# V in thirds over 128 partitions, ScalarE's copies swapped, and the last weight splits moved behind the lists

## The chip, the cores and the metric

The kernel runs on one core of one Trainium2 chip. The metric is the device time of one execution in microseconds (us), as the median of several runs; lower is better.

## The reference

Three layers in one kernel, all float32: an attention layer over 2 x 8 heads of 768 tokens, a top-2 mixture of 8 experts over the 1536 tokens, and a top-1 mixture with a skip. The change touches what is computed in the attention layer and between it and the first mixture's experts.

```python
def _attn_ref(q, k, v):                      # each (2, 8, 768, 64)
    block, window = (32, 16)
    k_sum = k.reshape(B, H, nb, block, D).max(axis=3)
    v_sum = v.reshape(B, H, nb, block, D).mean(axis=3)
    scores_l = scale * np.matmul(q, k.transpose(0, 1, 3, 2))
    mask_l = np.abs(pos[:, None] - pos[None, :]) < window
    scores_s = scale * np.einsum('bhsd,bhnd->bhsn', q, k_sum) + np.log(block)
    scores_all = np.concatenate([np.where(mask_l, scores_l, -1e9), scores_s], axis=-1)
    a = softmax(scores_all)
    return np.matmul(a, np.concatenate([v, v_sum], axis=2))

def _moe_ref(x, w_gate, w_noise, noise, w1, w2):
    noisy_logits = x @ w_gate + np.log1p(np.exp(x @ w_noise)) * noise
    top2 = np.argpartition(-noisy_logits, 2, axis=1)[:, :2]
    top2_w = softmax(noisy_logits[top2])
    for e in range(8):
        for k in range(2):
            mask = top2[:, k] == e
            out[mask] += top2_w[mask, k, None] * (np.maximum(x[mask] @ w1[e], 0.0) @ w2[e])
```

## The kernel before

The program is written engine by engine: SP issues the loads, PE (TensorE) multiplies, ACT (ScalarE), DVE (VectorE) and POOL (GpSimd) do the rest, each in an order written out by hand, with semaphores between them. An engine that waits holds everything behind it in its own order.

**Attention** works on 12 tiles of 128 tokens (6 per batch, `NT`), each in two steps of four heads (`NG = 2`, so 24 steps, `STEPS`). For a tile PE makes the scores of both steps (`scores`, L714) against a window of 96 keys and the 24 block maxima of the keys. DVE scales and masks them and takes the row maximum (`softmax`, L1562 and L1567). ACT takes the exponentials (`exponentials`, L1071). PE transposes them (`turn_p`, L725), ACT copies the transposed probabilities out of PSUM (`empty_pt`, L1078), and PE multiplies them with a window of V and the 24 block means of V (`times_v`, L742). DVE normalises a finished tile (`normalise`, L1574 to L1581) into `x_sb`, POOL stores it (`store_x`, L1324), PE transposes it (`do_job` of an "x" job, L676), ACT copies that (`empty_job`, L486, `xt_a`), and PE forms the router's logits (`router_logits`, L754). Every engine walks over the same step number s with lags: transposes at s - 2, P times V at s - 3, the x transposes at even steps from 6. On ACT a step is this, so that the copy of a step's probabilities stands at the beginning of the next step, behind the x copy (`PV_LAG = 3`):

```python
if 0 <= s - PV_LAG < STEPS:
    empty_pt(s - PV_LAG)
if 0 <= s - 1 < STEPS:
    exponentials(s - 1)
for job in at_step.get(s, []):
    empty_job(eng, job)
```

The first `times_v` of a tile waits until DVE has written `x_sb` of the tile before (semaphore `s_x`), since the accumulators are reused. The scores of a tile wait until the masks of the tile before are done (`s_masked`).

**Block means of V.** Raw V of a batch lies as 96 partitions of 8 tokens, in two halves of four tokens. POOL sums the first half (`value_sums`, L1316 and L1318), DVE the second (`value_sum`, L1550 and L1553), each in two additions; PE multiplies both with the matrix `mean` (L680, four matmuls, each shown twice by the profile). ACT copies the result to `vsum`, and POOL copies it into each of the eight windows of V (L1346), in between its copies of key windows (`window_of_keys`, L1303).

**Weights.** A set of weights is 8 pieces of 128 x 1024 numbers, loaded into `stage` by SP from the seventh tile on (`PIECE_TILE = 6`). Every product in the experts uses the weight rounded (`w_hi`) and the rest (`w_lo`). For the first set POOL rounds all pieces (`round_first`, L1329); DVE takes the rest of pieces 0 to 3 between attention steps (`split_first`, L1598, `SPLIT_AT`), and POOL itself the rest of pieces 4 to 7 after its last store (L1356).

**Routing** runs on DVE (`route`, L1639 to L1738) behind attention: softplus noise, top two, ranks of the tokens in their experts, then one-hot lists that PE multiplies, and the index lists (`index_lists`, L1757 to L1763). Then `first_mixture` starts: DVE clears a few buffers (L1774 to L1778), PE waits for that, runs twelve matmuls on nothing (`keep_warm`, L694), transposes the first gathered tokens (L815), which POOL gathers by an indirect DMA (L1430), and starts the first expert (L846).

**SP's queue** before the first tile: identity, keys of batch 0 in four transfers, the first of six query chunks, V in two halves, then tile by tile the windows of V, with the other queries, keys and V of batch 1 in between. Queries lie in rows of 1 KB. The third transfer of V waits for a free buffer (`VR = 3`).

## Time and profile before

| | |
|---|---|
| median of 3 runs | 688.26 us (687.83 to 688.34) |
| the profiled execution | 688.8 us, of which the span in the profile is 686.9 us |
| PE busy | 629.4 us (92%) |
| DVE, ACT, POOL busy | 369.5 (54%), 293.2 (43%), 247.3 us (36%) |
| mean granted TensorE clock | 0.946 of full speed |
| first expert matmul (L846) | 140.67 us after the span's start |
| attention, to the last logits | 105.0 us |
| routing and lists on DVE | 105.7 to 130.7 us |

The span's clock starts at the first instruction. All times of rows are in us from there. Matmuls of float32 appear as two records each. A busy engine is not necessarily the one that sets the end; for that the last wait of each step has to be read.

### The profile page before, as it was taken

To read this page: it belongs to the slowest core of one execution; us is meant where nothing else is said; L and a number is where in the kernel's file an instruction comes from. 1 tells how busy PE (TensorE), PEld (TensorE's weight loads), DVE (VectorE), ACT (ScalarE), POOL (GpSimd) and SP (SyncE) were. 2 spreads that over 40 slices of the span, in tenths; PEclk is the share of its full clock that TensorE was granted. 3 is DMA by queue.
4 is the path that set the end of the run, shared out by engine and by line. 5 is a ranking of instruction groups with operands and counts; after the bars stand their busy time and mean duration, and the time that the engine had idled before them with its cause. 6 is when DMAs were issued, how large, how long until landed. Compare 5 with 4: busy or idle time off the path is not lost.

```text
span 686.9 us, 13569 instructions
## 1 busy us (share of the span) xinstructions
PE 629.4 (92%) x4063; PEld 559.7 (81%) x4063; DVE 369.5 (54%) x711; ACT 293.2 (43%) x534; POOL 247.3 (36%) x231
## 2 busy tenths in 40 slices
PE   6788881699999999999999999999699999999994
PEld 6476771499999999999999999997478888888883
DVE  4564778655363545436354544630755669467541
ACT  2354750443253444335244432524254666546531
POOL 2552618220361816336170633606013223222130
PEclk9777996599999999999999999999799999999998
DMA  8985697236182654829265482798186859667321
GB/s 267 289 239 187 183 332 250 59 86 211 52 217 84 167 165 87 258 52 235 81 171 154 99 248 52 171 320 196 27 262 236 275 159 347 183 197 236 80 46 16
DMA packets 59380, 119.79 MB, mean 174 GB/s; under 512 B 13541, under 2 KB 16869, under 8 KB 58929
## 3 DMA queue, kind: packets, MB, share of 16 engines
q1 hardware_dynamic: 41168, 94.33, 42.9%
q0 software_dynamic: 14304, 23.93, 16.6%
q10 hardware_dynamic: 3840, 0.73, 0.5%
q8 instruction: 31, 0.51, 0.3%
q14 instruction: 37, 0.30, 0.1%
HBM read 103.48 MB, written 23.50 MB: 185 GB/s over the span
## 4 chain that ended last, share of the span: by engine, by line
PE 83%; DVE 5%; DMA 5%; SPq 2%; issue 2%; ACT 1%; POOLq 0%; DVEq 0%; ACTq 0%; POOL 0%
PE bank L960 22%; PE bank L852 21%; PE bank L846 21%; DMA q_ring<-in_q 3%; PE bank L835 2%; PE bank L815 2%; PE bank L742 2%; PE bank L976 2%; PE bank L754 2%; PE bank L694 2%; DMA xg<-x_moe,ix_take 1%; PE bank L714 1%; PE bank L725 1%; PE bank L764 1%; SPq L518 1%
## 5 line engine op out<-in xcount | busy, mean ns | idle before, releaser
L1589 DVE TENSOR_TENSOR w_lo<-stage,w_hi x120 | 141.6, 1222 | 22.9 <-ACT w_hi L1085 21.5
L1085 ACT CAST w_hi<-stage x120 | 119.7, 1050 | 9.4 <-PE bank L960 9.2
L852 PE MATMUL bank<-unit_hi,w_hi 128*128 128x416 f32 x256 | 92.6, 362 | 0.0
L846 PE MATMUL bank<-tok_hi,w_hi 128*128 128x416 f32 x256 | 90.5, 354 | 0.6 <-DVE tok_lo L1797 0.6
L852 PE MATMUL bank<-unit_lo,w_hi 128*128 128x416 f32 x256 | 90.2, 352 | 0.0
L1845 DVE SCALAR_TENSOR_TENSOR unit_lo<-bank,unit_hi 128x416 fp32r<-128x416 f32 x64 | 37.9, 592 | 96.9 <-ACT unit_hi L1186 96.9
L846 PE MATMUL bank<-tok_hi,w_lo 128*128 128x416 f32 x256 | 89.7, 351 | 0.0
L852 PE MATMUL bank<-unit_hi,w_lo 128*128 128x416 f32 x256 | 89.7, 350 | 0.0
L1186 ACT ACTIVATE unit_hi<-bank 128x416 fp32r<-128x416 f32 x64 | 33.2, 519 | 129.7 <-PE bank L846 129.7
L1396 POOL DMA_INDIRECT x_more<-more_out,ix_put x32 | 51.9, 1621 | 41.8 <-DVE more_out L1816 26.3
L1408 POOL DMA_INDIRECT x_moe<-rows_out,ix_put x32 | 55.2, 1726 | 9.8 <-issue 9.8
L846 PE MATMUL bank<-tok_lo,w_hi 128*128 128x416 f32 x256 | 58.5, 350 | 0.0
L1376 POOL COPY ix_take<-take_ix 128x4 int32 (+1 forms) x8 | 1.5, 186 | 135.8 <-PE bank L815 135.8
L846 PEld LDWEIGHTS bank<-tok_hi,w_hi 128*128 128x128 f32 x256 | 48.0, 188 | 1.6 <-issue 1.0
L852 PEld LDWEIGHTS bank<-unit_hi,w_hi 128*128 128x128 f32 x256 | 48.1, 188 | 1.0
L852 PEld LDWEIGHTS bank<-unit_hi,w_lo 128*128 128x128 f32 x256 | 48.3, 188 | 0.5
L846 PEld LDWEIGHTS bank<-tok_hi,w_lo 128*128 128x128 f32 x256 | 48.1, 188 | 0.4
L852 PEld LDWEIGHTS bank<-unit_lo,w_hi 128*128 128x128 f32 x256 | 48.0, 188 | 0.4
L846 PEld LDWEIGHTS bank<-tok_lo,w_hi 128*128 128x128 f32 x256 | 47.9, 187 | 0.5
L960 PE MATMUL bank<-w_hi,ht_hi 128*128 128x512 f32 x112 | 46.7, 417 | 0.0
L960 PE MATMUL bank<-w_hi,xt_hi 128*128 128x512 f32 x112 | 45.6, 407 | 0.5 <-ACT xt_hi L1229 0.5
L960 PE MATMUL bank<-w_lo,ht_hi 128*128 128x512 f32 x112 | 44.3, 395 | 0.0
(165 smaller groups left out, 1101.7 us busy)
## 6 DMA issues: line engine op xcount, KB each, us to landing
stage<-in_moe_w SPq DMA_DIRECT2D x128, 512.0 KB, 5.4
v_win<-in_v SPq DMA_DIRECT2D x24, 198.0 KB, 6.3
v_raw<-in_v SPq DMA_DIRECT2D x4, 792.0 KB, 12.2
x_moe<-rows_out SPq DMA_DIRECT2D x12, 260.0 KB, 3.8
kt<-in_k SPq DMA_DIRECT2D x8, 384.0 KB, 10.6
q_ring<-in_q SPq DMA_DIRECT2D x6, 512.0 KB, 10.4
x_att<-x_sb POOLq DMA_DIRECT2D x12, 256.0 KB, 5.4
x_part<-x_moe SPq DMA_DIRECT2D x4, 768.0 KB, 8.0
```

Source lines behind the costliest of these rows:

```text
L694: eng.matmul(ps[:], w_hi[0][:, 0, 0:P], w_hi[0][:, 0, :], start=True, stop=True)
L742: last = eng.matmul(ps_heads[part, h, 0:HD + 1], pt_sb[:, s % 2, i, part], v_win[:, (2 * t + half) % WR, h * VD:(h + 1) * VD], start=True, ...
L754: last = eng.matmul(ps_gate[:, t * cols:(t + 1) * cols], xt_a[t % 2][:, i, :], wgate1[:, i, :], start=(i == 0), stop=(i == DK - 1), skip_g ...
L846: last = eng.matmul(ps_unit[f % 2][:, 0:W], w, x, start=(i == 0), stop=(i == len(mine) - 1))
L852: last = eng.matmul(ps_out[chunk][:, 0:W], w[:, WC // 2 + f, chunk * P:(chunk + 1) * P], h[:, f % UNITS, :], start=(f == 0 and i == 0), st ...
L960: last = eng.matmul(ps[:], *every[i], start=(i == 0), stop=(i == len(every) - 1))
L1085: eng.copy(piece(w_hi[n % SETS], j), stage[:, j, :]).then_inc(s_hi, 1)
L1186: eng.activation(unit_hi[:, f % UNITS, :], ps_unit[f % 2][:, 0:W], ACT.Relu)\
L1396: eng.indirect_dma_start(more_dram, bass.IndirectOffsetOnAxis(ap=ix_put[0:rows, t:t + 1], axis=0), more_out[0:rows, t, :], None, bounds_ch ...
L1408: eng.indirect_dma_start(x1_dram, bass.IndirectOffsetOnAxis(ap=ix_put[0:rows, t:t + 1], axis=0), rows_out[0:rows, t, :], None, bounds_chec ...
L1589: eng.tensor_tensor(piece(w_lo[n % SETS], j), stage[:, j, :], piece(w_hi[n % SETS], j).bitcast(F32), ALU.subtract)\
L1845: eng.scalar_tensor_tensor(unit_lo[:, f % UNITS, :], ps_unit[f % 2][:, 0:W], 0.0, unit_hi[:, f % UNITS, :].bitcast(F32), ALU.max, ALU.subt ...
```

## The change

It has seven parts.

1. Raw V of a batch is loaded as three thirds of 128 partitions with two tokens each (`VJ, VI = 3, 2`), into one buffer per batch, so that SP waits for none. Batch 1's thirds are issued in tile 3 instead of 3 and 4.
2. DVE sums all of it in one instruction of 1584 elements, at steps 0 and 8 instead of 1 and 10, ahead of the next step's `softmax`; POOL sums nothing. PE multiplies with three matrices, so six matmuls instead of four; for batch 1 one step earlier.
3. The constants that only the casts of step 2 use (512 of 896 columns) are loaded by SP behind V instead of by ACT ahead of everything.
4. The queries are laid out on the host so that a chunk is one row of 4 KB per partition. The second chunk moves behind the first four windows, the keys of batch 1 one tile forward.
5. ACT copies the transposed probabilities in their own step, ahead of that step's x or V copy. POOL works by tiles: both V window copies, then both key windows.
6. The weight pieces are loaded two tiles earlier (`PIECE_TILE = 4`). POOL rounds pieces 0 to 3, ACT pieces 4 to 7, at steps 20, 22, 24 and 26. DVE splits pieces 0 to 3 two steps earlier (17 to 23).
7. DVE splits pieces 4 to 7 behind `index_lists` and ahead of `first_mixture`; POOL splits none. These pieces are the first expert's second layer.

On DVE at the start, up to the second tile's first mask (`v_part` is the sum of V, `s_sb` the masked scores), before:

```order
L1562 SCALAR_TENSOR_TENSOR s_sb<-bank,c_early 128x480
L1567 TENSOR_REDUCE nmax<-s_sb 128x4
L1562 SCALAR_TENSOR_TENSOR s_sb<-bank,c_early 128x480
L1567 TENSOR_REDUCE nmax<-s_sb 128x4
L1550 TENSOR_TENSOR v_raw<-v_raw 96x1056
L1553 TENSOR_TENSOR v_part<-v_raw 96x528
L1562 SCALAR_TENSOR_TENSOR s_sb<-bank,c_early 128x480
```

and with the change:

```order
L1539 SCALAR_TENSOR_TENSOR s_sb<-bank,c_early 128x480
L1544 TENSOR_REDUCE nmax<-s_sb 128x4
L1530 TENSOR_TENSOR v_part<-v_raw 128x1584
L1539 SCALAR_TENSOR_TENSOR s_sb<-bank,c_early 128x480
L1544 TENSOR_REDUCE nmax<-s_sb 128x4
L1539 SCALAR_TENSOR_TENSOR s_sb<-bank,c_early 128x480
```

The sum moves from behind the second mask to between the first and the second.

On ACT in the third and fourth tile (`pt_sb` are the transposed probabilities, `xt_a` the transposed x, `p_sb` the exponentials), before:

```order
L1078 COPY pt_sb<-bank 120x512
L1071 ACTIVATE p_sb<-s_sb,nmax 128x120 x4
L486 COPY xt_a<-bank 128x512
L1078 COPY pt_sb<-bank 120x512
L1071 ACTIVATE p_sb<-s_sb,nmax 128x120 x4
```

and with the change:

```order
L1058 ACTIVATE p_sb<-s_sb,nmax 128x120 x4
L1065 COPY pt_sb<-bank 120x512
L482 COPY xt_a<-bank 128x512
L1058 ACTIVATE p_sb<-s_sb,nmax 128x120 x4
L1065 COPY pt_sb<-bank 120x512
```

The copy of the probabilities and that of x have changed places.

On DVE between the lists and the first mixture (`put_ix` is the last of the lists, the memsets are the first of `first_mixture`), before:

```order
L1759 TENSOR_TENSOR empty<-c_late,count 128x128
L1762 TENSOR_SCALAR empty<-empty,c_late 128x128
L1763 TENSOR_TENSOR put_ix<-bank,empty 128x128
L1774 MEMSET rows_out 128x3x8
L1775 MEMSET more_out 128x36
```

and with the change:

```order
L1737 TENSOR_TENSOR empty<-c_late,count 128x128
L1740 TENSOR_SCALAR empty<-empty,c_late 128x128
L1741 TENSOR_TENSOR put_ix<-bank,empty 128x128
L1576 TENSOR_TENSOR w_lo<-stage,w_hi 128x1024 x4
L1752 MEMSET rows_out 128x3x8
L1753 MEMSET more_out 128x36
```

The four splits that POOL made beside the routing now stand here. The diff, cut to its core:

```diff
     parts["mask"] = mask
-    mean = np.zeros((P, NSUM), np.float32)
-    mean[p[:VP], p[:VP] * VTOK // BLOCK] = 1.0 / BLOCK
+    mean = np.zeros((P, VJ, NSUM), np.float32)
+    for j in range(VJ):
+        mean[p, j, j * (NSUM // VJ) + p // (BLOCK // VI)] = 1.0 / BLOCK
     parts["mean"] = mean
...
-        at_step = {2: [("v", 0, hh) for hh in range(2)], 12: [("v", 1, hh) for hh in range(2)]}
-
-        POOL_SUMS = {0: 0, 8: 1}
-        DVE_SUMS = {1: 0, 10: 1}
-        KEY_MAXIMA = {5: (0,), 6: (1,), 7: (2,), 8: (3,)}
+        at_step = {2: [("v", 0, hh) for hh in range(2)], 11: [("v", 1, hh) for hh in range(2)]}
+
+
+        SUMS = {0: 0, 8: 1}
+        KEY_MAXIMA = {4: (0,), 5: (1,), 6: (2,), 7: (3,)}
...
-        PIECE_TILE = 6
+        PIECE_TILE = 4
...
                     eng.wait_ge(s_score, NG * 2 * (n - QR + 1))
-                eng.dma_start(q_ring[:, n % QR], q[b, :, :, part * QC:(part + 1) * QC])\
+                eng.dma_start(q_ring[:, n % QR], q[b, part].rearrange("p (i n) -> p i n", i=PAIRS))\
                    .then_inc(s_q[n % QR], 16)
-            def load_values(b, part):
-                if 2 * b + part >= VR:
-                    eng.wait_ge(s_vp[(2 * b + part - VR) % 2], (2 * b + part - VR) // 2 + 1)
-                eng.dma_start(raw_of(b, part)[:], v[b].rearrange("(p j) c -> p j c", j=VTOK)
-                              [:, VHALF * part:VHALF * (part + 1), :]).then_inc(s_rawv[b, part], 16)
+            def load_values(b):
+                for j in range(VJ):
+                    eng.dma_start(v_raw[b][:, j, :], v[b, j * VI * P:(j + 1) * VI * P]
+                                  .rearrange("(p i) c -> p (i c)", i=VI)).then_inc(s_rawv[b, j], 16)
...
                 n, j = divmod(g, PIECES)
-                if n == 1 and j < PIECES // 2:
+                if n == 1:
                     eng.wait_ge(s_first, j + 1)
-                elif n == 1:
-                    eng.wait_ge(s_first_down, j - PIECES // 2 + 1)
                 elif n > 1:
...
             load_queries(0)
-            for part in range(2):
-                load_values(0, part)
+            load_values(0)
+            eng.dma_start(c_early[:, casts - early:], const[:, casts:]).then_inc(s_casts, 16)
             for t in range(NT):
-                if t == 2:
-                    load_queries(1)
                 for w in (2 * t, 2 * t + 1):
                     load_window(w)
-                if t == 2:
+                if t == 1:
+                    load_queries(1)
                     load_keys(1)
                 elif t == 3:
-                    load_values(1, 0)
                     load_queries(2)
-                elif t == 4:
-                    load_values(1, 1)
+                    load_values(1)
                     load_queries(3)
...
                     land(1)
-            for j in range(NT - PIECE_TILE, PIECES):
-                load_piece(j)
             land(0)
...
                     cols = slice(job[2] * VC, (job[2] + 1) * VC)
-                    for part in range(2):
-                        last = eng.matmul(ps[0:NSUM, 0:VC], c("mean")[0:VP], v_part[part][:, cols],
-                                          start=(part == 0), stop=(part == 1))
+                    for j in range(VJ):
+                        last = eng.matmul(ps[0:NSUM, 0:VC], c("mean")[:, j, :], v_part[:, j, cols],
+                                          start=(j == 0), stop=(j == VJ - 1))
                 last.then_inc(s_tr, 1)
...
                             if e == 0:
-                                eng.wait_ge(s_first_down, PIECES // 2)
+                                eng.wait_ge(s_first, PIECES)
                             else:
...
-            eng.dma_start(c_early[:], const[:, early:nconst]).then_inc(s_const, 16)
+            eng.dma_start(c_early[:, 0:casts - early], const[:, early:casts]).then_inc(s_const, 16)
             eng.dma_start(c_late[:, P:early], const[:, P:early]).then_inc(s_late, 16)
...
+            def round_first(j):
+
+                eng.wait_ge(s_loaded, j + 1)
+                eng.copy(piece(w_hi[0], j), stage[:, j, :]).then_inc(s_fhi_down, 1)
+
+            ROUND_AT = (20, 22, 24, 26)
             eng.preload_act_table_set("natural_log_exp_and_others")
             for s in range(LAST + 1):
-                if 0 <= s - PV_LAG < STEPS:
-                    empty_pt(s - PV_LAG)
                 if 0 <= s - 1 < STEPS:
                     exponentials(s - 1)
+                if 0 <= s - TURN_LAG < STEPS:
+                    empty_pt(s - TURN_LAG)
                 for job in at_step.get(s, []):
                     empty_job(eng, job)
+                if s in ROUND_AT:
+                    round_first(PIECES // 2 + ROUND_AT.index(s))
             eng.wait_ge(s_gt[0], NT)
...
-            def value_sums(b):
-
-                eng.wait_ge(s_rawv[b, 0], 16)
-                if b:
-                    for hh in range(2):
-                        eng.wait_ge(s_tr, job_at["v", b - 1, hh] + 1)
-                tokens = raw_of(b, 0)
-                eng.tensor_tensor(tokens[:, 0:2], tokens[:, 0:2], tokens[:, 2:4], ALU.add).then_inc(s_vadd, 1)
-                eng.wait_ge(s_vadd, b + 1)
-                eng.tensor_tensor(v_part[0][:], tokens[:, 0, :], tokens[:, 1, :], ALU.add)\
-                   .then_inc(s_vp[0], 1)
+            def sums_beside(w):
+
+                b = w // NWIN
+                for hh in range(2):
+                    wait_job(eng, ("v", b, hh))
+                if w >= WR:
+                    eng.wait_ge(s_pv, NG * ((w - WR) // 2 + 1))
+                eng.tensor_copy(v_win[0:NSUM, w % WR], vsum[b][:]).then_inc(s_vw, 1)
...
-            STORE_LAG, ROUND = 5, 14
-            AHEAD = WKR
-            for w in range(AHEAD):
+            ROUND = 6
+            for w in range(WKR):
                 window_of_keys(w)
-            for w in range(BATCH * NWIN):
-                b = w // NWIN
-                if w in POOL_SUMS:
-                    value_sums(POOL_SUMS[w])
-                if w + AHEAD < BATCH * NWIN:
-                    window_of_keys(w + AHEAD)
-                if w % NWIN < WR:
-                    for hh in range(2):
-                        wait_job(eng, ("v", b, hh))
-                    if w >= WR:
-                        eng.wait_ge(s_pv, NG * ((w - WR) // 2 + 1))
-                    eng.tensor_copy(v_win[0:NSUM, w % WR], vsum[b][:]).then_inc(s_vw, 1)
-                if w >= STORE_LAG and w % 2:
-                    store_x((w - STORE_LAG) // 2)
-                if ROUND <= w < ROUND + PIECES and w % 2 == 0:
-                    round_first((w - ROUND) // 2)
+            for t in range(NT):
+                for w in (2 * t, 2 * t + 1):
+                    if w % NWIN < WR:
+                        sums_beside(w)
+                for w in (2 * t + WKR, 2 * t + WKR + 1):
+                    if w < BATCH * NWIN:
+                        window_of_keys(w)
+                if t >= 2:
+                    store_x(t - 2)
+                if ROUND <= t < ROUND + PIECES // 2:
+                    round_first(t - ROUND)
             for t in (NT - 2, NT - 1):
                 store_x(t)
-            for j in range(PIECES // 2, PIECES):
-                round_first(j)
-                eng.wait_ge(s_fhi, j + 1)
-                eng.tensor_tensor(piece(w_lo[0], j), stage[:, j, :],
-                                  piece(w_hi[0], j).bitcast(F32), ALU.subtract).then_inc(s_first_down, 1)
...
-
-                eng.wait_ge(s_rawv[b, 1], 16)
+                for j in range(VJ):
+                    eng.wait_ge(s_rawv[b, j], 16)
                 if b:
...
                         eng.wait_ge(s_tr, job_at["v", b - 1, hh] + 1)
-                tokens = raw_of(b, 1)
-                eng.tensor_tensor(tokens[:, 0:2], tokens[:, 0:2], tokens[:, 2:4], ALU.add)\
-                   .then_inc(s_vadd_d, 1)
-                eng.wait_ge(s_vadd_d, b + 1)
-                eng.tensor_tensor(v_part[1][:], tokens[:, 0, :], tokens[:, 1, :], ALU.add)\
-                   .then_inc(s_vp[1], 1)
+                eng.tensor_tensor(v_part[:], v_raw[b][:, :, 0:VROW], v_raw[b][:, :, VROW:2 * VROW],
+                                  ALU.add).then_inc(s_vp, 1)
...
-                eng.wait_ge(s_fhi, j + 1)
-                for hh in range(2):
-                    eng.wait_ge(s_vp[hh], BATCH)
+                if j < PIECES // 2:
+                    eng.wait_ge(s_fhi, j + 1)
+                else:
+                    eng.wait_ge(s_fhi_down, j - PIECES // 2 + 1)
                 eng.tensor_tensor(piece(w_lo[0], j), stage[:, j, :],
...
-            SPLIT_AT = (19, 21, 23, 25)
+            SPLIT_AT = (17, 19, 21, 23)
             steps = [0]
...
                 if s == 2:
+                    eng.wait_ge(s_casts, 16)
                     eng.tensor_copy(before_b[:], c("before")).then_inc(s_cast, 1)
...
                     then(eng.tensor_copy(column_h[:], c("column")))
-                if s in DVE_SUMS:
-                    value_sum(DVE_SUMS[s])
+                if s in SUMS:
+                    value_sum(SUMS[s])
                 if s in SPLIT_AT:
...
             index_lists(0)
+            for j in range(PIECES // 2, PIECES):
+                split_first(j)
             first_mixture()
...
         laid[n] = pairs.reshape(BATCH, P, PAIRS, SEQ)
+    chunks = laid["q"].reshape(BATCH, P, PAIRS, QCHUNKS, QC).transpose(0, 3, 1, 2, 4)
+    laid["q"] = chunks.reshape(BATCH, QCHUNKS, P, PAIRS * QC)
     by_token = inputs["v"].transpose(0, 2, 1, 3)
```

## Rows read from the trace of the kernel before

**Rows 1.** The page: granted TensorE clock in 40 slices, tenths of full speed

```profile
PEclk9777996599999999999999999999799999999998
```

**Rows 2.** Windows: stretch, length, busy PE, PEld, DVE, ACT, POOL; clock, DMA share, GB/s

```profile
24.00:32.00 8.00, 6.72 (x76) 5.43 (x76) 2.11 (x6) 5.18 (x16) 5.77 (x11) 0.50 1.05 305
68.00:104.00 36.00, 31.19 (x517) 27.79 (x509) 25.00 (x45) 23.68 (x66) 14.66 (x24) 1.00 0.79 261
```

**Rows 3.** Timeline of PE in attention: start us, us, engine, line, operation [idle before]

```profile
15.42 1.05 PE L714 MATMUL bank<-k_win,q_ring 64*64 64x120 f32 x32
21.36 2.74 PE L680 MATMUL bank<-v_part,c_early 96*24 96x264 f32 x8 [3.43 <-DVE v_part L1553]
27.48 1.88 PE L714 MATMUL bank<-k_win,q_ring 64*64 64x120 f32 x32
39.06 1.59 PE L714 MATMUL bank<-k_win,q_ring 64*64 64x120 f32 x32 [1.01 <-DMA q_ring<-in_q]
...
61.10 3.71 PE L680 MATMUL bank<-v_part,c_early 96*24 96x264 f32 x8
67.65 1.05 PE L714 MATMUL bank<-k_win,q_ring 64*64 64x120 f32 x32
...
89.31 1.05 PE L714 MATMUL bank<-k_win,q_ring 64*64 64x120 f32 x32
```

**Rows 4.** Timeline of DVE in the routing, and of POOL beside it

```profile
105.74 1.22 DVE L1639 TENSOR_TENSOR score<-z_sp,noise_sb 128x96 f32<-128x96 f32 x1 [3.19 <-ACT z_sp L1105]
107.00 0.26 DVE L1641 TENSOR_TENSOR score<-bank,score 128x96 f32<-128x96 f32 x1
110.43 0.90 DVE L1673 CAST top_f<-top_ix 128x24 f32<-128x24 uint32 x1
111.76 2.28 DVE L1690 TENSOR_TENSOR mask_b<-hot 128x96 bf16<-128x96 f32 x1
113.97 1.00 DVE L1692 TENSOR_SCALAR first_f<-top_f 128x24 f32<-128x24 f32 x1
115.59 1.91 DVE L1707 TENSOR_SCALAR den<-den 128x12 f32<-128x12 f32 x1
...
111.38 2.56 POOL L1356 TENSOR_TENSOR w_lo<-stage,w_hi 128x1024 fp32r<-128x1024 f32 x1
```

**Rows 5.** Timeline of DVE, its sums of V

```profile
18.22 2.07 DVE L1550 TENSOR_TENSOR v_raw<-v_raw 96x1056 f32<-96x1056 f32 x1 [2.77 <-DMA v_raw<-in_v]
53.34 1.24 DVE L1550 TENSOR_TENSOR v_raw<-v_raw 96x1056 f32<-96x1056 f32 x1
54.62 0.70 DVE L1553 TENSOR_TENSOR v_part<-v_raw 96x528 f32<-96x528 f32 x1
```

**Rows 6.** Windows of the first transfers, columns as in rows 2

```profile
8.00:10.00 2.00, 2.00 (x16) 1.87 (x14) 1.65 (x3) 0.00 (x0) 0.27 (x1) 1.00 1.10 400
14.00:16.00 2.00, 2.00 (x36) 1.83 (x38) 1.41 (x3) 1.77 (x6) 0.63 (x1) 1.00 0.96 220
```

**Rows 7.** Timeline of PE, ACT and DVE in one attention tile at full clock

```profile
74.04 0.65 PE L725 MATMUL bank<-c_late,p_sb 128*120 128x128 f32 x4
...
77.86 0.69 PE L742 MATMUL bank<-v_win,pt_sb 120*64 120x65 f32 x16 [0.73 <-ACT pt_sb L1078]
...
76.73 0.59 ACT L486 COPY xt_a<-bank 128x512 f32<-128x512 f32 x1 [1.58 <-PE bank L676]
77.22 0.59 ACT L1078 COPY pt_sb<-bank 120x512 f32<-120x512 f32 x1
...
76.59 0.69 DVE L1581 TENSOR_TENSOR x_sb<-bank,rden 128x512 f32<-128x512 f32 x1
```

**Rows 8.** Timeline of DVE's splits of weights, and of PE's warm-up before the experts

```profile
83.87 1.81 DVE L1598 TENSOR_TENSOR w_lo<-stage,w_hi 128x1024 fp32r<-128x1024 f32 x1
89.29 1.22 DVE L1598 TENSOR_TENSOR w_lo<-stage,w_hi 128x1024 fp32r<-128x1024 f32 x1
...
131.52 4.61 PE L694 MATMUL bank<-w_hi 128*128 128x512 f32 x12 [2.24 <-DVE bank L1777]
```

31 lines of the change are left out of this document (13 added, 18 removed).

## The prediction

> **What bounds the kernel now.** I read the page's clock line and the windows of the first 150 us, then the chain of waits there, then the engines' timelines. The diff touches only what comes before the first expert layer, so all from the first expert matmul on is taken as unchanged and the sum lies in the first 141 us. TensorE (PE) carries the chain through attention. The reader is to see its two speeds: the clock line has 7 tenths in the three slices from 17 to 69 us [rows 1]; between 68 and 104 us PE has its full clock, in 24 to 32 us 0.50 of it, the lower of its two levels, 1.2 GHz [rows 2]. The starts of the score matmuls are the mileposts [rows 3]: second tile 15.42, third 27.48, fifth 39.06, eighth 67.65, twelfth 89.31 us. From the eighth on a tile takes (89.31-67.65)/4 = 5.42 us; the three from the fifth to the eighth took 28.59. Behind attention VectorE (DVE) computes the routing alone, and five of its small instructions take 0.9 to 2.3 us there, beside one of 96 elements at 0.26, while GpSimd (POOL) works on the weights [rows 4].
>
> **The change part by part.** The mileposts give the terms.
>
> *Start, up to the third tile.* DVE waits for V until 18.2 us [rows 5], and PE's V matmuls start at 21.36 [rows 3]. V (1.62 MB) passes in a stretch of 220 GB/s over 96 partitions; keys over 128 partitions came at 400 [rows 6]. At 220 V costs 7.4 us, at 400 4.1. The constants for the casts (0.26 MB, 0.7 us) also leave the stretch ahead of V. So V lands between 14.2 (both gains) and 18.2 (none); I take 15, near the fast row, because the thirds have the keys' 128 partitions. The new sum is one instruction of 1584 elements in place of 1056 and then 528, which take 1.24 and 0.70 us with POOL idle [rows 5], so 1.24 + 0.54 = 1.8. It now stands ahead of the second group's mask (0.7), and PE's second scores wait for that mask: 15 + 1.8 + 0.7 = 17.5. Scores, transposes and filler follow, 2.5 us as from 15.42 to the pause at 21.36 - 3.43 = 17.93 [rows 3]: 20.0. Then six V matmuls in place of four: a pass of four took 3.71 us at the low clock [rows 3], so six take 5.6 there and 2.8 at full. They end at 22.8 to 25.6. From their end (24.10) to the third scores 3.4 us passed before; the same gives 26.2 to 29.0. I take 26.8, nearer the full clock, since PE's pause is now only from about 15.5 to 17.5: **-0.7** (ends -2.1, with V at 14.2, and +4.7, with V at 18.2 and the low clock).
>
> *Third to fifth tile*, 11.58 us. With V faster and 0.8 MB less queued ahead of it, the third query chunk lands 4 us or more earlier, and PE's 1.01 us behind it go [rows 3]. The block maxima of the second keys come one step earlier and fill DVE, so I count no more: **-1.0** (0 to -2.0).
>
> *Fifth to eighth tile*, 28.59 us. Three tiles at 5.42 are 16.3, DVE's sum in front of a mask is 1.24 + 0.70 = 1.9 [rows 5], the V matmuls at full clock 1.9; that is 20.1, so 8.5 go to the low clock. Afterwards: three tiles at 4.9 (next term) 14.7, the sum 1.8, the V matmuls 2.8, together 19.3. The loss to the clock is what I know least: between 0 and the same 8.5. Of PE's pauses in this stretch the one behind queries goes and that behind ACT shrinks; that behind the sum stays. I take 6, nearer to before: 25.3, **-3.3** (-9.3 to -0.8).
>
> *The four tiles at full clock.* Here the swap on ScalarE (ACT) tells. PE's transposes of an even step are done at 74.04 + 0.65 = 74.69, but ACT empties them only at 77.22, because the copy of x stands first and waits for PE's own x transposes until 76.73; P times V starts at 77.86, having waited 0.73 [rows 7]. With the swap ACT is done before 76. What is late next is the normalisation: this P times V may not start before DVE has written x_sb, at 76.59 + 0.69 = 77.28. So it starts at 77.33, 0.53 earlier, and a tile takes 4.89. PE's own work is 5.42 - 0.73 = 4.7 a tile; DVE is busy 25.00 of 36 us, 3.8 a tile with its splits, ACT 23.68, 3.6 [rows 2], and 4.8 with a rounding if that takes what a split takes, 1.2 [rows 8]. All stay just under 4.89. Four tiles: **-2.1** (to 0, if roundings push an exponential).
>
> *The drain to the routing* has one more such wait, 0.5, and one of ACT's four roundings may stand before the last x copies, 0.3: **-0.2** (-0.5 to +0.8).
>
> *Routing.* The five slow instructions take 1.22 + 0.90 + 2.28 + 1.00 + 1.91 = 7.3 us. mask_b ends at 114.04 just as POOL's subtract of 111.38 does, at 113.94 [rows 4]: DVE is held behind POOL. With POOL idle they take at most 0.26 each, 1.3: **-6.0** (-6.4 to -5).
>
> *The splits behind the lists.* Four of DVE's 1024-element subtracts now stand between the lists and the memsets for which PE's twelve warm-up matmuls, at 131.52, wait [rows 8]. Nothing covers them; they in turn cover the gathers. Four by 1.22 are **+4.9** (4.5 to 7.2, the last by 1.81 each, the split that ran beside a POOL cast [rows 8]). POOL issues its four gathers just then; a gather's issue reads only a few indices, so I stay at 1.22. The next set's last four pieces load later for it, but their use is a whole expert round away.
>
> *At nothing:* queries in rows of 4 KB. The first queries, in rows of 1 KB, passed in the stretch of 400 GB/s [rows 6]. Thirds of 0.54 MB in place of halves of 0.81: DMA share is 0.96 to 1.10 with several transfers queued [rows 6], so a third costs its bytes. The Trainium skill (DMA: Bandwidth & Descriptors, "Rules for kernel authors") asks for 1 MiB or more per DMA and speaks against this part; with the page's fixed 2 us for the one transfer more, the sum would be an estimated -6.4. The share on these rows speaks against it.
>
> **Sum:** -0.7 -1.0 -3.3 -2.1 -0.2 -6.0 +4.9 = -8.4. The profiled execution took 688.8 us (span 686.9), so 680.4; it lies 0.5 above the median of the runs, 688.26, so I say **679.9**.
>
> **Rivals.**
> *The clock stays up.* Without the low level between the fifth and eighth tile that term is -9.3 and the time 679.9 - 6.0 = 673.9. For it: between 68 and 104 us PE was busy 31.19 of 36 us and kept its clock [rows 2], and 4.7 in 4.89 is denser. Against: DVE's sum still makes PE wait.
>
> *The clock falls as before.* The pause before the second scores brings the low level at the start (+2.2 on that term) and again later (-0.8 for -3.3): 679.9 + 4.7 = 684.6. For it: the low window of 24 to 32 us [rows 2] followed a pause of 3.43 us [rows 3].
>
> *The splits are held behind POOL's gathers,* 1.81 each: +2.3, 682.2. For it: mask_b and the 1.81 [rows 4, 8]. Against: no row shows a gather's issue holding DVE. The Trainium skill (SBUF — State Buffer, "Who interferes with whom") has this rule for a VectorE instruction with two SBUF inputs against a GpSimd one that reads SBUF, the later waiting for the whole of the earlier.
>
> *V is no faster in thirds* (18.2): 679.9 + 3.2 = 683.1.
>
> *The end on the other side: V is late for DVE's in-order queue.* The sum stands ahead of the second mask, so until all three thirds are in, masks, exponentials and PE stand, and each microsecond of V beyond 15 is one of the whole, at the low clock. That is the second rival's 684.6 plus the delay; it decides from V at 15 + 3.7 = 18.7 us, hardly later than now, and at 21 the kernel takes 690.6. For it: V is waited for as a whole before the second mask. Against: it was there at 18.2 behind more bytes.
>
> **How the numbers follow.** Forecast 0.40, clock up 0.16, clock as before 0.20, splits held 0.10, V no faster 0.08, V late 0.06. The range runs from the clock that stays up to the second rival with held splits or a late V in part: 673.5 to 686.0. A measurement of this kernel tells 0.2% (1.4 us) from no change. All but the last rival are faster by more, with a little off for two of them together: 0.90; within 0.2% 0.04; slower 0.06.
>
> **What would show it.** Right: V's sum on DVE starts at 14 to 16 us; third scores near 27, eighth near 63, twelfth near 82; a tile in 4.9 us with P times V waiting for DVE, not ACT; mask_b and den at 0.3 or less; four w_lo of 1.2 between put_ix and the memsets; the first expert matmul some 8 us earlier than before. Wrong: a V sum after 18 us; a clock of 0.50 through most of 22 to 60 us; w_lo behind the lists at 1.8; a tile above 5.2; a first expert matmul less than 3 us earlier.

## The result and the profile after

The changed kernel takes 678.92 us (median; 673.55 to 685.43 over 13 executions), the kernel before beside it 687.49. The medians differ by 8.6 us, where the prediction said 8.4; the ratio is 0.9892, 95% interval 0.9854 to 0.9931, which is 7.4 us. Both kernels vary by about 1% from one execution to the next, the slower ones mostly at a lower mean clock (0.952 to 0.972 for the changed kernel); the ratios leave out executions more than 1.5% above the fastest of the same kernel, such as one of 722.98 us among the six of warm_held. The profiled execution took 673.55 us (span 671.2) and is its quickest, so the 15.7 us between the two profiled spans are more than the change is worth at the median. Where a stretch is compared below, I also use the traces of experiments whose code is the same there.

The page's clock line of the changed kernel, against [rows 1]:

```profile
PEclk9999975999999999999999999999699999999998
```

Windows of the changed kernel (stretch, length, busy PE, PEld, DVE, ACT, POOL; clock, DMA share, GB/s), against [rows 2, 6]:

```profile
8.00:10.00 2.00, 0.48 (x5) 0.24 (x3) 1.54 (x2) 0.00 (x0) 0.72 (x3) 1.00 1.04 426
14.00:16.00 2.00, 0.68 (x7) 0.44 (x5) 1.94 (x2) 0.67 (x3) 0.00 (x0) 1.00 1.08 250
24.00:32.00 8.00, 6.30 (x141) 5.08 (x137) 6.13 (x11) 5.08 (x15) 7.47 (x15) 1.00 1.04 344
40.00:48.00 8.00, 6.10 (x99) 4.86 (x95) 5.99 (x10) 5.04 (x15) 2.22 (x6) 1.00 0.91 271
```

The clock is 1.00 throughout attention, up to 88 us. Before, it stood at 0.50 from 24 to 32 us [rows 2]. By SP's order the 250 GB/s from 14 to 16 us are windows of V, which go onto 96 partitions; V itself is in by then.

Timeline of PE: the mileposts, against [rows 3] (start, us, [idle before]):

```profile
16.58 1.05 PE L701 MATMUL bank<-k_win,q_ring 64*64 64x120 f32 x32 [1.90 <-DVE s_sb L1539]
19.02 2.85 PE L667 MATMUL bank<-v_part,c_early 128*24 128x264 f32 x12
24.60 1.05 PE L701 MATMUL bank<-k_win,q_ring 64*64 64x120 f32 x32 [0.17 <-issue]
34.90 1.38 PE L701 MATMUL bank<-k_win,q_ring 64*64 64x120 f32 x32 [0.78 <-DVE s_sb L1539]
41.89 1.05 PE L701 MATMUL bank<-k_win,q_ring 64*64 64x120 f32 x32 [1.64 <-DVE s_sb L1539]
54.56 1.05 PE L701 MATMUL bank<-k_win,q_ring 64*64 64x120 f32 x32
74.98 1.05 PE L701 MATMUL bank<-k_win,q_ring 64*64 64x120 f32 x32
```

Second, third, fifth, sixth, eighth and twelfth scores, with the V matmuls between the first two. Third 24.60 against 27.48, fifth 34.90 against 39.06, eighth 54.56 against 67.65, twelfth 74.98 against 89.31.

Timeline of DVE, then of POOL and PE behind the lists, against [rows 4, 5, 8]:

```profile
14.06 1.81 DVE L1530 TENSOR_TENSOR v_part<-v_raw 128x1584 f32<-128x1584 f32 x1 [0.68 <-DMA v_raw<-in_v]
91.69 0.26 DVE L1617 TENSOR_TENSOR score<-z_sp,noise_sb 128x96 f32<-128x96 f32 x1 [3.32 <-ACT z_sp L1100]
95.76 0.26 DVE L1668 TENSOR_TENSOR mask_b<-hot 128x96 bf16<-128x96 f32 x1
96.73 0.17 DVE L1685 TENSOR_SCALAR den<-den 128x12 f32<-128x12 f32 x1
109.83 0.29 DVE L1741 TENSOR_TENSOR put_ix<-bank,empty 128x128 int32<-128x128 f32 x1
110.27 4.63 DVE L1576 TENSOR_TENSOR w_lo<-stage,w_hi 128x1024 fp32r<-128x1024 f32 x4
...
111.54 2.01 POOL L1411 DMA_INDIRECT rows_in<-x_att,take_ix  x1 [0.30 <-issue]
116.11 0.95 POOL L1411 DMA_INDIRECT rows_in<-x_att,take_ix  x1 [0.30 <-issue]
...
115.23 4.70 PE L681 MATMUL bank<-w_hi 128*128 128x512 f32 x12 [6.53 <-DVE bank L1755]
124.48 0.45 PE L833 MATMUL bank<-tok_hi,w_hi 128*128 128x416 f32 x1 [0.58 <-DVE tok_lo L1775]
```

Routing and lists, from score to the end of put_ix, take 18.4 us against 24.9 (105.74 to 130.69). Then four splits in 4.63, and only then the warm-up. From the first expert matmul on the two traces differ little: 671.2 - 124.5 = 546.7 us here, 686.9 - 140.7 = 546.2 before.

### The profile page after: what moved, and what is told of

Read it like the earlier page. It is cut to its first block, busy times and chain, and to the rows that moved or that the text cites. A ratio compares the mean times of both kernels' runs of the same rounds, so it can differ in the third digit from the quotient of the medians.

```text
span 671.2 us, 13575 instructions
## 1 busy us (share of the span) xinstructions
PE 618.5 (92%) x4071; PEld 551.4 (82%) x4071; DVE 367.0 (55%) x713; ACT 297.0 (44%) x538; POOL 230.3 (34%) x219
## 4 chain that ended last, share of the span: by engine, by line
PE 85%; DVE 6%; DMA 3%; issue 2%; ACT 1%; SPq 1%; POOLq 0%; DVEq 0%; POOL 0%; ACTq 0%
PE bank L947 22%; PE bank L839 22%; PE bank L833 22%; PE bank L822 2%; PE bank L802 2%; PE bank L963 2%; PE bank L729 2%; PE bank L681 2%; PE bank L741 2%; PE bank L701 1%; PE bank L712 1%; DMA xg<-x_moe,ix_take 1%; DMA v_raw<-in_v 1%; PE bank L919 1%; DVE col_val L1728 1%
```

## The experiments

Each experiment was run beside the kernel before, on the same chip. Microseconds between two kernels are differences of these ratios times 686.

### Where DVE's routing instructions lost their time

**splits_pool**: the changed kernel with the last four subtracts on POOL.

```diff
 # POOL, behind the last store_x
+for j in range(PIECES // 2, PIECES):
+    eng.wait_ge(s_fhi_down, j - PIECES // 2 + 1)
+    eng.tensor_tensor(piece(w_lo[0], j), stage[:, j, :],
+                      piece(w_hi[0], j).bitcast(F32), ALU.subtract).then_inc(s_first_down, 1)
 # DVE, behind index_lists(0)
-for j in range(PIECES // 2, PIECES):
-    split_first(j)
```

> The changed kernel with the last four subtracts back on POOL, behind its last store of x, so beside the routing; the roundings stay on ACT. If POOL's subtract holds DVE's small instructions (the theory): those routing instructions that fall beside the four subtracts (some 2.6 us each, about 90 to 100 us) take 0.9 to 2.3 again, the stretch from the router's score to put_ix grows from 18.4 by 3 to 6 us, and the memsets come 4.6 sooner behind put_ix: the first expert matmul stands within -1.6 and +1.5 us of the changed kernel's. If the slow instructions of the kernel before came from something else (its POOL casts, or the place in the program): the stretch stays at 18.4, the first expert matmul comes 4.6 us sooner, and the whole takes some 674.5.

Measured: 683.28 us, ratio 0.9941 (0.9907 to 0.9975). Timeline of its POOL and DVE:

```profile
95.50 9.26 POOL L1344 TENSOR_TENSOR w_lo<-stage,w_hi 128x1024 fp32r<-128x1024 f32 x4
100.95 3.93 DVE L1624 TENSOR_TENSOR score<-z_sp,noise_sb 128x96 f32<-128x96 f32 x1 [6.39 <-ACT z_sp L1103]
104.91 0.26 DVE L1626 TENSOR_TENSOR score<-bank,score 128x96 f32<-128x96 f32 x1
```

POOL's four subtracts end at 104.76; DVE's 96-element score, which takes 0.26 alone, starts at 100.95 and ends at 104.88. All that follow are at full speed. So POOL holds DVE, and the whole growth of the stretch (22.1 us instead of 18.4) is this one instruction. The Trainium skill (SBUF — State Buffer, "Who interferes with whom") has the later instruction wait for the whole of the earlier one; here it waited for the next of the run as well, which started at 102.4. By the rows this kernel should equal the changed one: from score to the first expert matmul (133.80) it takes 32.9 us against 32.8, 3.7 lost in the routing and 3.6 won back behind the lists. The ratios put it 3.4 above, with intervals that overlap, and this rest I can't settle.

**before_splits**: the kernel before with the subtracts moved and POOL's roundings left.

```diff
 # POOL, behind the last store_x
 for j in range(PIECES // 2, PIECES):
     round_first(j)
-    eng.wait_ge(s_fhi, j + 1)
-    eng.tensor_tensor(piece(w_lo[0], j), stage[:, j, :],
-                      piece(w_hi[0], j).bitcast(F32), ALU.subtract).then_inc(s_first_down, 1)
 # DVE, behind index_lists(0)
+for j in range(PIECES // 2, PIECES):
+    split_first(j)
```

> The kernel before with this part of the change alone: the last four subtracts go from POOL to DVE, behind the lists; POOL keeps their four roundings beside the routing. If only POOL's subtracts held DVE: the five slow instructions fall to 0.3 or less, score to put_ix from 24.95 to some 19, four subtracts of 1.2 follow, and the first expert matmul comes 1 us or so sooner (time -1.3). If its casts hold DVE too: two or three of the five stay slow, and the whole is 1 to 3 us slower than the kernel before.

Measured: 686.9 us, ratio 1.0029 (0.9995 to 1.0064). The timeline of its POOL and DVE shows that the cast holds DVE as well, to the end of the run of four at 100.35:

```profile
96.37 3.98 POOL L1329 CAST w_hi<-stage 128x1024 fp32r<-128x1024 f32 x4
98.73 1.74 DVE L1637 TENSOR_TENSOR score<-z_sp,noise_sb 128x96 f32<-128x96 f32 x1 [3.19 <-ACT z_sp L1105]
118.90 4.63 DVE L1595 TENSOR_TENSOR w_lo<-stage,w_hi 128x1024 fp32r<-128x1024 f32 x4 [0.25 <-DVE put_ix L1761]
```

Four casts alone are over before the second slow instruction comes, so score to the end of put_ix takes 19.9 us, 5.0 less than before, and the subtracts give 4.4 back (memsets 4.83 behind put_ix, 0.45 before). **This part alone is worth nothing that can be measured.** The routing's gain and the splits' price nearly cancel: score to the first expert matmul takes 34.7 us against 34.9.

### What ScalarE's order carries

**swap_undone**: the changed kernel with the old order.

```diff
-if 0 <= s - 1 < STEPS:
-    exponentials(s - 1)
-if 0 <= s - TURN_LAG < STEPS:
-    empty_pt(s - TURN_LAG)
+if 0 <= s - PV_LAG < STEPS:
+    empty_pt(s - PV_LAG)
+if 0 <= s - 1 < STEPS:
+    exponentials(s - 1)
```

> The changed kernel with ScalarE's old order (probabilities of three steps back emptied first, then the exponentials, and the x copy ahead of the next emptying). If the swap carries what was predicted (0.53 a tile at full clock): the P times V matmuls of an even step again wait some 0.6 to 0.7 for ACT's pt_sb, the tiles from the eighth to the twelfth take 5.3 to 5.5 instead of 5.1 on average, and the whole is 3 to 6 us above the changed kernel (some 682 to 685). If DVE sets the pace of a tile anyway (rival): the tile stays at 5.1, the wait only changes its name, and the time is that of the changed kernel, 679 within a microsecond or two.

Measured: 687.4 us, ratio 1.0019 (0.9991 to 1.0047): the whole gain of the change is gone, more than the 682 to 685 expected. PE's waits in its timeline:

```profile
72.25 0.69 PE L729 MATMUL bank<-v_win,pt_sb 120*64 120x65 f32 x16 [0.73 <-ACT pt_sb L1065]
84.03 0.69 PE L729 MATMUL bank<-v_win,pt_sb 120*64 120x65 f32 x16 [1.67 <-ACT pt_sb L1065]
90.39 0.69 PE L729 MATMUL bank<-v_win,pt_sb 120*64 120x65 f32 x16 [1.67 <-ACT pt_sb L1065]
96.30 0.69 PE L729 MATMUL bank<-v_win,pt_sb 120*64 120x65 f32 x16 [1.67 <-ACT pt_sb L1065]
```

Tiles take 5.42 us again, the 0.73 of [rows 7], instead of 4.95. Three times the wait is 1.67: ACT's rounding of a weight piece, which takes 1.05, now stands between the x copy and the emptying that PE waits for (83.39). In its ACT timeline, ahead of the first of the three:

```profile
81.96 0.59 ACT L482 COPY xt_a<-bank 128x512 f32<-128x512 f32 x1 [1.56 <-PE bank L663]
82.44 1.05 ACT L1083 CAST w_hi<-stage 128x1024 fp32r<-128x1024 f32 x1
```

This P times V waits 0.26 in the changed kernel. Six waits of 0.73 are 0.47 longer, 2.8 us; three of 1.67 are 1.41 longer, 4.2: together an estimated 7.0 of the 8.7 lost. So the roundings on ACT are affordable only in the new order.

**before_swap**: the kernel before with that order alone (the same edit the other way round).

> The kernel before with ScalarE's new order alone. Undoing it in the changed kernel cost 8 us where 3 to 6 were expected, so the order may carry more than a wait of 0.53 a tile. If it does so by itself: the tiles from the eighth to the twelfth go from 5.42 to 4.9, those before them have shorter pauses and keep the clock more often, and the time falls by 4 to 8 us, to some 680. If it needs the other parts (V in time, the block maxima earlier; rival): the late tiles take 4.9, which is 2 us, the early ones stay as they were, and the time is 683 to 684.

Measured: 681.92 us, ratio 0.9950 (0.9912 to 0.9989), 3.4 us, between what its two expectations say. The eighth to the eleventh scores stand at 59.99, 64.94, 69.88 and 74.83, so 4.95 a tile, also without the other parts. Earlier tiles keep waits that the order doesn't touch, 3.10 us behind queries and 1.83 behind DVE's sum, with the clock at 0.50 from 40 to 44 us.

### V: partitions, and its place in DVE's queue

**v_96**: the changed kernel, each third as 96 and 32 partitions.

```diff
-for j in range(VJ):
-    eng.dma_start(v_raw[b][:, j, :], v[b, j * VI * P:(j + 1) * VI * P]
+for p0, p1 in ((0, 96), (96, P)):
+    for j in range(VJ):
+        eng.dma_start(v_raw[b][p0:p1, j, :], v[b, j * VI * P + VI * p0:j * VI * P + VI * p1]
...
-    eng.wait_ge(s_rawv[b, j], 16)
+    eng.wait_ge(s_rawv[b, j], 32)
```

> The changed kernel with each third of V as two transfers, partitions 0 to 95 first (all three thirds), then the other 32; the bytes are the same. If the 96 partitions of the kernel before held its V at 220 GB/s (the theory): the 1.2 MB on 96 partitions pass at 220 to 270 GB/s in some 5 us, V's sum on DVE starts at 16 to 17.5 instead of 14 to 15.7 us, PE's pause grows by as much, and the whole takes 1 to 5 us more than the changed kernel. If the length of the rows set the rate (rival; they stay at 4.2 KB here): 400 GB/s throughout, and the sum starts as before within 0.5 us.

Measured: 685.28 us, ratio 0.9983 (0.9946 to 1.0021), 6.2 us above the changed kernel. Its window and its V sum:

```profile
14.00:16.00 2.00, 0.95 (x9) 0.71 (x7) 0.00 (x0) 0.95 (x4) 0.00 (x0) 1.00 1.03 223
```

```profile
17.86 1.81 DVE L1532 TENSOR_TENSOR v_part<-v_raw 128x1584 f32<-128x1584 f32 x1 [4.20 <-DMA v_raw<-in_v]
```

The same bytes in the same row length pass at 223 GB/s, DMA share 1.03, where the changed kernel has 400 and more up to 14 us. The partitions set the rate, not the rows. The smaller transfers (0.4 MB) don't either: the halves of 0.81 MB of the kernel before, also onto 96 partitions, pass at 220 [rows 6]. The sum starts 3.8 us later than in the changed kernel's trace, the third scores 6.4 (31.01).

**v_late**: the changed kernel, V's three transfers behind the first four windows and the second queries.

```diff
-load_values(0)
...
 if t == 1:
     load_queries(1)
+    load_values(0)
     load_keys(1)
```

> The changed kernel with V's thirds issued behind the first four windows and the second queries, so some 4.7 us later (windows of 0.2 MB at 230 GB/s, queries of 0.5 MB at 400). By the prediction's last rival the whole delay shows at the third tile (29 to 30 instead of 24.6 us), PE pauses for 6 us and its clock falls to 0.50 behind that: 5 us of delay and 2 to 6 of clock, so 686 to 690. If the next tiles win it back, since DVE has slack once V is there (rival): less than 3 us remain, 680 to 682.

Measured: 685.84 us, ratio 0.9985 (0.9948 to 1.0021). Its PE in the timeline, and the page's clock line:

```profile
22.37 1.88 PE L701 MATMUL bank<-k_win,q_ring 64*64 64x120 f32 x32 [7.30 <-DVE s_sb L1539]
```

```profile
PEclk9898995799999999999999999999699999999998
```

DVE waits 6.1 us for V and sums at 19.9; PE stands for 7.30, and its clock is 0.50 from 20 to 24 us. Third scores at 31.87, 7.3 late; the twelfth at 84.68, 6.9 behind warm_held's and q_1k's 77.8. By the ratios 6.4 us remain: nearly nothing is won back.

**sum_behind**: the changed kernel, DVE's first sum one step later, behind the second mask.

```diff
-SUMS = {0: 0, 8: 1}
+SUMS = {1: 0, 8: 1}
```

> The changed kernel with DVE's first sum of V one step later, behind the second group's mask. If the in-order queue is what stops PE (its second scores waited 1.90 for that mask in the changed kernel's trace, up to 2.94 in a sibling's): the second scores start at some 14.5 instead of 16.6 us, the V matmuls at 17 instead of 19, the third scores near 22.5 instead of 24.6, and the clock falls in fewer executions: 2 to 5 us off, some 675. If V's own arrival sets the third tile (rival): the third scores come within 0.5 us of the changed kernel's and the time stays at 679.

Measured: 675.49 us, ratio 0.9811 (0.9757 to 0.9865), 5.6 us better than the changed kernel, though the two intervals touch. Second scores at 15.40 without the wait of 1.90, third at 23.41, where 22.5 was expected: 1.2 us sooner than in the changed kernel's trace (24.60) and up to 2.4 sooner than in two others with the same code there (25.75, 25.83). So the in-order queue was the price of the sum's new place; the rows show 1.2 to 2.4 us of it, the rest of the 5.6 is not shown.

**q_1k**: the changed kernel with the queries in rows of 1 KB.

```diff
-q[b, part].rearrange("p (i n) -> p i n", i=PAIRS)
+q[b, :, :, part * QC:(part + 1) * QC]
```

> The changed kernel with the queries again in rows of 1 KB instead of 4 KB. Predicted at nothing, from 400 GB/s in the stretch where the first queries passed in such rows: the GB/s in the stretches of the queries stay near 400, V's sum starts at 14 to 15.7 us, and the time is that of the changed kernel, 679 within 1.5 us. If short rows pass slower (rival): V's sum comes 0.5 us or more later than 15.7, and the time is 1 to 4 us above.

Measured: 681.32 us, ratio 0.9884 (0.9815 to 0.9954), that of the changed kernel. By the 1.6 MB of keys queued ahead of them the first queries pass between 7 and 9 us: that stretch carries 390 GB/s, 415 in the changed kernel's trace. V's sum starts at 14.14 against 14.06, the third scores at 24.67 against 24.60. So the rows cost 0.1 us at most there; the ratio's interval alone would leave room for the rival's 1 to 4 us.

### PE's pauses and its clock

**before_filled**: the kernel before with filler on PE where it paused.

```diff
-IDLE = {0: 16, 1: 8, 2: 8, STEPS + 3: 8}
+IDLE = {0: 16, 1: 8, 2: 34, 7: 8, 11: 10, STEPS + 3: 8}
```

> The kernel before with 44 more filler transposes on PE: 26 ahead of its first V matmuls, where it paused 3.43 us, 8 ahead of the fifth tile's scores (pause 1.01), 10 ahead of the seventh's (1.35). They write a part of a bank that nothing reads. If PE's pauses bring the clock down (the theory behind the low level between 22 and 66 us): the granted clock stays at 1.00 from 16 to 56 us, the eighth tile's scores come at 59 to 62 instead of 67.7, and the whole takes some 680. If the clock falls for other reasons (rival): the clock line stays as it was, filler at half the clock costs 0 to 2 us more, and the time is 686 to 688.

Measured: 682.27 us, ratio 0.9929 (0.9900 to 0.9958), 4.9 us for work that computes nothing. Its windows:

```profile
24.00:32.00 8.00, 6.05 (x108) 5.14 (x112) 3.62 (x9) 4.90 (x15) 6.02 (x12) 0.79 1.05 300
40.00:48.00 8.00, 6.96 (x128) 6.17 (x117) 5.76 (x10) 3.94 (x11) 3.60 (x10) 1.00 0.99 264
```

0.79 and 1.00, where the profiled execution of the kernel before had 0.50 for the whole of both stretches, the first in [rows 2], the second here:

```profile
40.00:48.00 8.00, 6.66 (x56) 5.50 (x50) 3.66 (x8) 1.81 (x6) 2.50 (x5) 0.50 0.67 214
```

The expectation of 1.00 throughout was missed from 24 to 32 us. The eighth scores come at 59.23 instead of 67.65, but most of these 8.4 us are not the filler's: that profiled execution was a poor one for the clock. before_splits has the same code as the kernel before up to the routing, without filler, and its windows and eighth scores are:

```profile
40.00:44.00 4.00, 4.00 (x34) 3.84 (x31) 1.55 (x4) 0.00 (x0) 0.50 (x1) 0.50 0.83 235
44.00:48.00 4.00, 3.69 (x61) 3.06 (x60) 3.29 (x6) 3.24 (x10) 1.64 (x5) 0.76 0.68 166
60.66 1.05 PE L714 MATMUL bank<-k_win,q_ring 64*64 64x120 f32 x32
```

Against this trace the eighth scores come 1.4 us sooner. What shows that the pauses bring the clock down is the ratio, whose interval over 12 executions is clear of 1, and the stretch from 40 to 48 us at 1.00 where both traces without filler fall to 0.50. The 12 executions spread over 5.5 us, the 29 of the kernel before beside them over 10.8. That it also falls to a varying degree behind the same pause is seen in siblings of the changed kernel, whose code is the same here. In q_1k's timeline and window:

```profile
41.96 1.64 PE L701 MATMUL bank<-k_win,q_ring 64*64 64x120 f32 x32 [1.64 <-DVE s_sb L1539]
```

```profile
40.00:48.00 8.00, 6.36 (x75) 5.78 (x72) 4.44 (x8) 3.01 (x9) 1.74 (x5) 0.64 0.82 259
```

The wait of 1.64 is the same as in the changed kernel's trace; there the clock stayed at 1.00, here it is 0.64. Fifth to eighth tile take 22.4 us instead of 19.7. The same holds in splits_warm, splits_pool, warm_held, v_late and sum_behind, with 22.1 to 22.7, while v_96 kept its clock and took 19.3: six of the eight traces with this code and this wait lose some of the clock.

### Splits beside the warm-up, and a version that beats both

**splits_warm**: the changed kernel, memsets first.

```diff
 # DVE, first_mixture
 eng.memset(out_t[:], 0.0).then_inc(S["yt"], DK)
+for j in range(PIECES // 2, PIECES):
+    split_first(j)
 # DVE, behind index_lists(0)
-for j in range(PIECES // 2, PIECES):
-    split_first(j)
```

> The changed kernel with the memsets ahead of the last four subtracts, so that PE's twelve warm-up matmuls run beside the subtracts. If the 4.6 us of subtracts lay bare on the path: memsets follow put_ix within 0.2, the warm-up starts at some 110.9 instead of 115.2, and the first expert matmul comes 3.7 to 4.5 us sooner, some 675 in all. If the gathers bound it (their issue on POOL took 2.0 instead of 1.1 beside the subtracts, and the last ended at 117.1): PE waits for rows_in and at most 1 to 2 us come back, some 677.5.

Measured: 679.44 us, ratio 0.9901 (0.9865 to 0.9937): no gain. PE in its timeline:

```profile
114.73 5.04 PE L681 MATMUL bank<-w_hi 128*128 128x512 f32 x12 [2.24 <-DVE bank L1755]
125.69 1.45 PE L802 MATMUL bank<-c_late,rows_in 128*128 128x128 f32 x8 [3.47 <-DMA rows_in<-x_att,take_ix]
```

The warm-up starts 0.8 behind put_ix as meant, but the third gather lands at 125.7, 6.4 after its issue had ended. Its issue, and ahead of it the loads of the next set on SP:

```profile
116.17 3.77 SPq L562 DMA_DIRECT2D stage<-in_moe_w  x4
117.37 1.93 POOL L1411 DMA_INDIRECT rows_in<-x_att,take_ix  x1 [0.31 <-issue]
```

Each split releases a 512 KB load of the next set, and 2.1 MB of loads share the DMA engines with the gathers (384 GB/s at a share of 1.02 from 122 to 124 us).

**warm_held**: the same, with those loads behind the gathers.

```diff
 # SyncE, load_piece of the second set
 eng.wait_ge(s_first, j + 1)
+if j == PIECES // 2:
+    eng.wait_ge(s_take[PARTS - 1], 16)
```

> The kernel with the memsets ahead of the last four subtracts, plus one wait on SyncE: the next set's last four pieces load only once the first four gathers have landed. If those 2.1 MB of loads delayed the gathers (the third landed at 125.7 us, 6.4 after its issue had ended): PE no longer waits for rows_in, put_ix to first expert matmul goes from 14.6 to some 10.5 us, and the whole stands 4 us below the changed kernel, some 675. If gathers were slow beside the subtracts themselves, since POOL's issue took 1.9 instead of 1.0 (rival): PE's wait for rows_in stays above 2 us and the time is 678 to 679.

Measured: 675.07 us, ratio 0.9824 (0.9770 to 0.9877). PE waits for no gather, and 10.3 us lie between put_ix and the first expert matmul instead of splits_warm's 14.6 (14.4 in the changed kernel), though POOL's second and third issue still take 1.7 and 1.9. The loads were the cause.

**best**: all of it, with both sums and the key maxima behind odd masks and ACT's roundings behind attention.

```diff
-SUMS = {0: 0, 8: 1}
-KEY_MAXIMA = {4: (0,), 5: (1,), 6: (2,), 7: (3,)}
+SUMS = {1: 0, 9: 1}
+KEY_MAXIMA = {5: (0, 1), 7: (2, 3)}
 # ACT
-ROUND_AT = (20, 22, 24, 26)
...
 eng.activation(z_sp[:], z_exp[:], ACT.Ln, bias=1.0).then_inc(s_z, 1)
+for j in range(PIECES // 2, PIECES - 1):
+    round_first(j)
...
 weights(0, GROUPS[0][0])
+round_first(PIECES - 1)
 store_gates(0, GROUPS[0][0])
```

The roundings at the steps of `ROUND_AT` are gone, and the edits of warm_held are in.

> A candidate from what the runs showed, on the changed kernel: both sums of V, and the second keys' block maxima two by two, behind the mask of an odd step; ACT's last four roundings behind the attention's end; the memsets ahead of the last four subtracts; SyncE loads the next pieces only once the first four gathers have landed. If DVE's order in front of a mask, the roundings in front of exponentials and the collision of loads with gathers are what was left: third scores near 23.4 us, fifth near 33, twelfth near 73, score to first expert matmul 28 to 29 us instead of 32.8, and 666 to 671 in all. If the gathers come no earlier without the loads (rival): PE waits for rows_in again behind the warm-up, and the gain over the 675.5 of the kernel with the first sum moved is 1 to 2 us.

Measured: 666.75 us (665.16 to 669.19), ratio 0.9709 (0.9656 to 0.9761), 20 us below the kernel before and 12.6 below the changed kernel. Its PE, late in the timeline, and one window:

```profile
71.46 1.05 PE L703 MATMUL bank<-k_win,q_ring 64*64 64x120 f32 x32
106.17 4.38 PE L683 MATMUL bank<-w_hi 128*128 128x512 f32 x12 [2.24 <-DVE bank L1757]
115.65 0.45 PE L835 MATMUL bank<-tok_hi,w_hi 128*128 128x416 f32 x1 [0.55 <-DVE tok_lo L1779]
```

```profile
40.00:48.00 8.00, 7.36 (x97) 5.23 (x96) 4.48 (x9) 4.68 (x13) 3.40 (x9) 1.00 0.94 290
```

The clock is 1.00 up to 88 us. No wait for a mask is left in front of scores. The spread of its six executions is 4 us, where the changed kernel's 13 had 12; with before_filled this speaks for pauses as a source of the spread too. The moved key maxima and roundings were not tried by themselves. Behind the first expert matmul this trace takes 551.1 us, 4.4 more than the changed kernel's, and why isn't shown.

## Why the prediction was right, and where its steps were off

**Start, -0.7:** it was -2.9. V landed at 14.0 in the profiled execution (15.3 and 15.7 in splits_warm and swap_undone) where I took 15, and the V matmuls ran at the full clock, 2.85 us. Both lay at the fast end of my range, which was -2.1. The end was set 0.8 too tight, mostly since it kept 3.4 us from the V matmuls to the third scores; 2.7 passed (21.87 to 24.60). In splits_warm and splits_pool the sum started at 15.3 and 15.2, and the term was -1.7. v_96 confirms the reason: 128 partitions.

**Third to fifth, -1.0:** -1.3 (34.90 - 24.60 = 10.3 against 11.58). The wait behind queries is gone, and PE waits 0.78 for masks behind DVE's maxima instead.

**Fifth to eighth, -3.3:** this is the term that was mis-sized. The 19.3 without clock loss was right, 19.66. The loss of 6 was not: it was 0 in the profiled execution and 2.4 to 3.0 in four other traces of this code (q_1k, splits_warm, splits_pool, warm_held), so against the 28.59 of before the term is -5.9 to -6.5 there and -8.9 in the profiled case. I held it near the 8.5 of before because DVE's sum still makes PE wait. It does, by 1.64 us. The fault lies further back: I took the 8.5 lost in one execution for the kernel's loss. In before_splits, with the same code there, the stretch takes 22.07 us (38.59 to 60.66), so the kernel before loses anything from 2 to 8.5 there. Against that trace the change gains from 2.4 us to nothing in this stretch, and what it gives at the median is open.

**Four tiles, -2.1:** -1.2 in the profiled execution. Two tiles took the 4.9 forecast, as their mileposts 54.56, 59.51 and 64.45 show, and P times V waits 0.25 or so instead of 0.73. It starts 0.10 behind the end of x_sb, as forecast:

```profile
63.04 0.69 DVE L1558 TENSOR_TENSOR x_sb<-bank,rden 128x512 f32<-128x512 f32 x1
63.83 0.69 PE L729 MATMUL bank<-v_win,pt_sb 120*64 120x65 f32 x16 [0.25 <-issue]
```

The other two took 5.27 and 5.26, because DVE's splits beside POOL's casts take 1.81 instead of 1.22 there and stand in front of a normalisation. I had the 1.81 row and used it only for the lists. The swap as a whole was much more than this term: my steps priced the wait it takes away now, 0.53 a tile, not what the old order would cost once ACT also rounds (swap_undone).

**Drain, -0.2:** +0.3 in the profiled execution (16.7 us from the twelfth scores to score, 16.4 before). ACT's rounding in step 22 delays the exponentials, and PE waits for them:

```profile
79.30 1.05 ACT L1083 CAST w_hi<-stage 128x1024 fp32r<-128x1024 f32 x1
80.25 1.25 ACT L1058 ACTIVATE p_sb<-s_sb,nmax 128x120 f32<-128x120 f32 x4
81.55 0.65 PE L712 MATMUL bank<-c_late,p_sb 128*120 128x128 f32 x4 [1.39 <-ACT p_sb L1058]
```

Behind this wait the clock fell in q_1k and splits_pool, and the drain took 21.8 us there. My range for it, -0.5 to +0.8, left this case out: +5.4 in two of the five traces that share the code. In q_1k, 9.0 us of span above the profiled execution, it makes 5.1 and the fifth to eighth tile 2.8.

**Routing, -6.0:** -6.5. POOL holding DVE is shown by splits_pool. **Splits, +4.9:** +4.4, at 1.16 each (memsets 0.45 behind put_ix before, 4.74 behind it now, and with it a start of the warm-up 4.3 later). The rival that they are held behind the gathers is refuted: it is the gathers' issue that is held.

**At nothing:** the queries' rows, as q_1k shows. The thirds too: with V at over 400 GB/s in transfers of half a megabyte, no cost of staying below the threshold in the Trainium skill (DMA: Bandwidth & Descriptors, "Rules for kernel authors") shows here.

**The rivals.** The clock that stays up, 673.9, is the profiled execution, 673.55. The forecast fits the median: the steps missed by -2.2 to -1.0, -0.3, -2.6 to -3.2, +0.9, +0.5 to +5.6, -0.5 and -0.5, which in part cancel. So the hit within 1 us is partly luck; what holds of the mechanism is V's rate, the wait of P times V, POOL's hold on DVE and the price of the splits. The late V was the right mechanism, as v_late shows. With V at 19.8 the time equals that of before, where the prediction had the point at 18.7. V no faster was priced too low, at +3.2: v_96, whose sum starts at 17.9, is 6.2 above the changed kernel; in its trace PE pauses for 5.43 us and the clock is at 0.50 from 20 to 24 us behind that.

The change's parts don't add. The splits' move alone is nothing, the swap alone 3.4 us; yet taking the swap out of the whole costs 8.7, and V's partitions 6.2.

## What to carry to other kernels

On an in-order queue, ask of each added instruction what stands behind it. A sum or a rounding ahead of the instruction that feeds the bottleneck can cost its whole length or most of it, behind it next to nothing (sum_behind, swap_undone). Where the bottleneck's clock depends on its pauses, a pause costs more than its length and may bring spread as well. Then one profiled execution is not the kernel: look at a stretch in several traces with the same code before pricing it (28.59 and 22.07 us for the same three tiles). And moving work out of a shadow can release transfers that collide with what the path waits for next (splits_warm against warm_held).
